# Retention core of a three-layer kernel: head-on-partition inputs, gapped scans, k decay on GpSimd, two sets of score banks

## The chip, the core and the metric

The kernel runs on one core of a Trainium2 chip. That core has five engines with instruction queues of their own: PE (TensorE, matrix products), DVE (VectorE), ACT (ScalarE), POOL (GpSimd) and SP (SyncE, which here only issues transfers). They meet through semaphores. The time is that of one execution on the device in microseconds (us); lower is better.

## What is computed

Three layers in a row: a linear recurrence with decay (4 sequences, 8 heads, 768 tokens, head dimension 48), then two layers of mixture of experts. The change touches only the recurrence:

```python
state = np.zeros((B, H, D, D), dtype=np.float32)
for t in range(S):
    kt, vt, rt, wt = (k[:, :, t], v[:, :, t], r[:, :, t], w[:, :, t])
    cur = np.einsum('bhd,bhe->bhde', u[None] * kt, vt)
    y[:, :, t] = np.einsum('bhd,bhde->bhe', rt, state + cur)
    state = wt[:, :, :, None] * state + np.einsum('bhd,bhe->bhde', kt, vt)
```

The first expert layer sends each of the 3072 tokens (rows of 384 numbers) to one of 8 experts, `out[mask] = gate_w * (relu(x @ w1[e]) @ w2[e])`; the second sends each to two experts. w lies between 0.8 and 0.95.

## The kernel before

The recurrence goes in 24 steps, one for each chunk of 128 tokens of a sequence (6 chunks for each of 4 sequences, all 8 heads at once). `batches` (L318) makes of the first three sequences a hardware loop of six written-out steps, and writes the last six out behind it. What each engine does, and in which order, is written by hand in its own block; a step of number g takes its operands from the buffers of step g+1 or g-1 where the text below says so.

The recurrence within a chunk is turned into products: `rest` holds, for each head dimension, the product of the decays behind a token, and `grow` the reciprocal of the products from a token on. k times `rest` is `k_dec`, r times `grow` is `r_dec`. The scores of a head are k_dec by r_dec, masked with `causal` (L719); the output is scores by v (L1083) plus r_dec by the state from the chunks before (L1080), into one bank of PSUM; DVE adds the term of u, `bonus_v`, and writes `y_tok` (L741). The state for the next chunk is k_tok (k_dec transposed, L1061, and copied by ACT, L562) by v (L1070) plus the old state (L734), times the total decay (L736). The input comes with tokens on the 128 partitions, so PE transposes w, k and r of the next chunk (`turn`, L1018: twelve transposes of two heads each) into three PSUM banks, and DVE's `decay_step` (L676) reads them there: four scans for `rest` (L685), one for each pair of heads, a reciprocal, k_dec (L691), four scans for `grow` (L694), r_dec (L699).

The order of a step g on the engines:
- PE: scores (L1053), transposes of k_dec (L1061), `turn` for g+1 (L1026), state products (L1070), transposes of y_tok of step g-1 (L1034), output products (L1080 and L1083), gate products (L1042, after ACT has copied the transposed rows, L552).
- DVE: mask (two halves, L719), bonus (L724), `decay_step` of g+1, state_sum, state, y_tok.
- POOL: rk = r*k (L434), ruk = rk*u (L437), bonus_v (L441), each 128 x 384.
- ACT: k_tok, the copies for the gate, and the store of y_tok.
- SP: for chunk g+3, four loads of 192 KB with 48 floats in a row (L332, L334) once step g's output is done, and a store of zeros into the output (L345).

The expert layers (from L446, L570, L776, L1095 on) begin when the last y_tok is stored; their lines are the same before and after, but for their numbers.

## Time and profile before

| what | value |
|---|---|
| median of 3 runs | 1128.05 us |
| lowest and highest of them | 1124.4 and 1131.2 us |
| span of the profiled execution, first to last instruction | 1121.9 us |
| busy share of the span: PE, DVE, POOL, ACT | 88%, 50%, 32%, 26% |
| the recurrence, from the first transpose on PE to the last y_tok | about 8 to 200 us |
| the rest: routing and the first expert layer, gate, routing and the second | about 200 to 1120 us |

For the profiled execution the records give the span alone and no time of its own, so the span stands for it; the median is 6.15 us longer. The busy share of the whole span says nothing about the recurrence, which is 17% of it: there PE and DVE are both nearly always busy, which the stretches in the rows below show. PEclk is the granted clock of TensorE, 1.00 for 2.4 GHz and 0.50 for 1.2 GHz. Rows of a line give its count, its busy time, and the mean time of one.

### The profile page before, as it was taken

The numbers are of one execution on the slowest core, as the hardware profiler recorded it, in microseconds if no ns is written. First come the engines' busy times: TensorE is split into PE (matmuls) and PEld (weight loads), VectorE is DVE, ScalarE is ACT, GpSimd is POOL, SyncE is SP. The second block draws the span as 40 slices with busy tenths as digits, with TensorE's granted clock in tenths as the row PEclk, the third lists the DMA queues.
The fourth block names the chain that finished last, engine by engine and source line by source line (L and its number), as shares of the span: only waits on it lengthen the run. The fifth ranks groups of instructions, "written<-read, shape, count | busy, mean of one in ns | idle before, by whom it ended". The sixth has DMA issues, their size and how long they took to land.

```text
span 1121.9 us, 25632 instructions
## 1 busy us (share of the span) xinstructions
PE 984.0 (88%) x6268; PEld 883.5 (79%) x6269; DVE 564.7 (50%) x1120; ACT 294.0 (26%) x462; POOL 360.5 (32%) x440
## 2 busy tenths in 40 slices
PE   6999999359999999959138999999999999999995
PEld 5988998248888889848027888889889888889884
DVE  5998999754333233314885335353533535353331
ACT  1111111214222222214123233242422324242220
POOL 4333333324222222210253334243433424343222
PEclk9998999569999999988559999999999999999998
DMA  8667564331111111133304525252252425222222
GB/s 144 154 146 168 135 155 126 119 101 70 43 42 42 42 39 38 39 99 103 114 14 153 144 42 147 36 154 42 33 164 35 148 42 152 45 35 41 38 43 35
DMA packets 149662, 97.17 MB, mean 87 GB/s; under 512 B 114224, under 2 KB 140592, under 8 KB 149616
## 3 DMA queue, kind: packets, MB, share of 16 engines
q1 hardware_dynamic: 124096, 60.00, 19.2%
q0 software_dynamic: 14400, 31.55, 13.7%
q10 hardware_dynamic: 11120, 5.09, 1.6%
q8 instruction: 20, 0.33, 0.1%
q14 instruction: 26, 0.21, 0.1%
HBM read 71.79 MB, written 24.82 MB: 86 GB/s over the span
## 4 chain that ended last, share of the span: by engine, by line
PE 68%; DVE 9%; issue 2%; DMA 2%; ACT 1%; POOLq 0%; POOL 0%; DVEq 0%; SPq 0%; ACTq 0%
PE ps L1167 19%; PE ps L1169 19%; PE ps L1168 19%; PE ps L1188 6%; PE ps L1162 2%; DVE row_mix L940 1%; PE ps L1103 1%; PE ps L1114 1%; DVE low_hot L864 1%; DVE slot_cmp L875 1%; DMA stage<-in_moe_w_dram 1%; DMA sx<-moe_rows,src_now 1%; PE ps L1123 1%; DVE high_is L860 1%; DVE x_lo L947 1%
## 5 line engine op out<-in xcount | busy, mean ns | idle before, releaser
L952 DVE SCALAR_TENSOR_TENSOR hid_lo<-ps,hid_hi 128x512 fp32r<-128x512 f32 x154 | 106.3, 690 | 313.8 <-ACT hid_hi L632 309.9
L1167 PE MATMUL ps<-w_hi,hid_hi 128*128 x616 | 215.0, 349 | 5.0 <-issue 3.5
L1167 PE MATMUL ps<-w_hi,x_hi 128*128 (+1 forms) x462 | 199.1, 431 | 20.1 <-DVE x_lo L947 12.9
L1168 PE MATMUL ps<-w_lo,hid_hi 128*128 x616 | 207.9, 337 | 0.0
L1169 PE MATMUL ps<-w_hi,hid_lo 128*128 x616 | 207.8, 337 | 0.0
L1168 PE MATMUL ps<-w_lo,x_hi 128*128 (+1 forms) x462 | 185.4, 401 | 0.0
L1169 PE MATMUL ps<-w_hi,x_lo 128*128 (+1 forms) x462 | 185.3, 401 | 0.0
L627 ACT ACTIVATE h_tok<-ps 128x512 f32<-128x512 f32 x154 | 92.2, 599 | 314.6 <-PE ps L1169 275.4
L498 POOL DMA_INDIRECT out_dram<-sy,dst_now x52 | 92.7, 1783 | 211.9 <-DVE sy L963 202.8
L632 ACT ACTIVATE hid_hi<-ps 128x512 fp32r<-128x512 f32 x154 | 91.9, 597 | 250.2 <-PE ps L1188 245.0
L1167 PEld LDWEIGHTS ps<-w_hi,hid_hi 128*128 128x128 f32 x616 | 116.3, 189 | 10.1 <-issue 6.6
L1167 PEld LDWEIGHTS ps<-w_hi,x_hi 128*128 128x128 f32 x462 | 88.3, 191 | 42.3 <-issue 27.1
L1168 PEld LDWEIGHTS ps<-w_lo,hid_hi 128*128 128x128 f32 x616 | 116.3, 189 | 3.2
L1169 PEld LDWEIGHTS ps<-w_hi,hid_lo 128*128 128x128 f32 x616 | 116.0, 188 | 0.0
L1169 PEld LDWEIGHTS ps<-w_hi,x_lo 128*128 128x128 f32 x462 | 88.5, 192 | 21.7
L1168 PEld LDWEIGHTS ps<-w_lo,x_hi 128*128 128x128 f32 x462 | 88.9, 192 | 14.6
L1188 PE MATMUL ps<-ident,h_tok 128*128 128x128 f32 x616 | 92.4, 272 | 5.2 <-ACT h_tok L627 5.2
L1188 PEld LDWEIGHTS ps<-ident,h_tok 128*128 128x128 f32 x616 | 76.1, 140 | 12.7 <-ACT h_tok L627 7.4
L477 POOL DMA_INDIRECT sx<-moe_rows,src_now x55 | 56.3, 1023 | 44.1 <-POOL src_now L474 42.4
L495 POOL DMA_INDIRECT moe_rows<-sy,dst_now x25 | 26.4, 1055 | 137.0 <-DVE sy L960 137.0
L613 ACT ACTIVATE w_hi<-stage 128x1536 f32 (+1 forms) x40 | 58.7, 1478 | 5.8 <-DMA stage<-in_moe_w_dram 5.7
L945 DVE CAST x_hi<-ps 128x384 fp32r<-128x384 f32 x79 | 43.7, 553 | 31.6 <-PE ps L1162 31.6
(195 smaller groups left out, 1273.7 us busy)
## 6 DMA issues: line engine op xcount, KB each, us to landing
stage<-in_moe_w_dram SPq DMA_DIRECT2D x20, 1536.0 KB, 12.1
out_dram<-zeros SPq DMA_DIRECT2D x25, 192.0 KB, 3.7
w_in<-in_w_dram SPq DMA_DIRECT2D x24, 192.0 KB, 2.7
k_in<-in_k_dram SPq DMA_DIRECT2D x24, 192.0 KB, 3.3
r_in<-in_r_dram SPq DMA_DIRECT2D x24, 192.0 KB, 4.1
v_in<-in_v_dram SPq DMA_DIRECT2D x24, 192.0 KB, 4.2
x_rows<-y_tok ACTq DMA_DIRECT2D x24, 192.0 KB, 3.3
stage<-moe_rows SPq DMA_DIRECT2D x6, 768.0 KB, 4.6
```

The lines of the kernel that those rows point to most:

```text
L477: pool.indirect_dma_start(out=sx[u][:, 0:width], out_offset=None, in_=rows, in_offset=bass.IndirectOffsetOnAxis(ap=src_now[u][:, :].bitcas ...
L495: pool.indirect_dma_start(out=y_dram, out_offset=where, in_=sy[u][:, :], in_offset=None)\
L498: pool.indirect_dma_start(out=out, out_offset=where, in_=sy[u][:, 0:C], in_offset=None, compute_op=ALU.add).then_inc(s_scatter[l][u], 16)
L613: act.activation(hi[:, bass.ds((n % 2) * WSZ + at, HALF)], raw[:, at:at + HALF], ACT.Copy)\
L627: act.activation(h_tok[:, half * FC // 2:(half + 1) * FC // 2, :], h_ps[half], ACT.Copy)\
L632: act.activation(hid_hi[:, half * FC // 2:(half + 1) * FC // 2, :], hT_ps[half], ACT.Relu)\
L945: dve.tensor_copy(x_hi[:, :, :], sxT_ps).then_inc(s_xhi[l], 1)
L952: dve.scalar_tensor_tensor(hid_lo[:, part, :], hT_ps[half], 0.0, hid_hi[:, part, :], ALU.max, ALU.subtract).then_inc(s_hlo[l], 1)
L1167: pe.matmul(out_ps, hi, w_hi[:, bass.ds(at, width)], start=first, stop=False)
L1168: pe.matmul(out_ps, hi, w_lo[:, bass.ds(at, width)], start=False, stop=False)
L1169: return pe.matmul(out_ps, lo, w_hi[:, bass.ds(at, width)], start=False, stop=final)
L1188: last = pe.transpose(hT_ps[half][:, m, :], h_tok[:, half * FC // 2 + m, :], ident[:, :])
```

## The change

The host lays the inputs out in three arrays. w_T and kr_T have the head dimension first: 48 rows for the even heads (partitions 0 to 47) and 48 for the odd ones (64 to 111), tokens along the row, so `turn` and its three PSUM banks go; rkv keeps r, k and v with tokens on partitions, for rk, bonus_v and the products with v. SP issues five loads for a chunk where it issued four: two of 96 KB for w, two of 192 KB for k and r, one of 576 KB; 1152 KB in all for 768 KB.

`w_in` gets a gap of one zero between the four pairs of heads. A scan over all 516 columns, state = w*state + seed, starts anew in a gap, since the seed tile holds 1 there (or the reciprocal of the total) and 0 elsewhere: one scan (L717) takes the place of the four of L685, one (L729) that of the four of L694. Both inputs of each lie in SBUF. k_dec moves from DVE to POOL (L443), where rk and ruk of step g+1 now also come ahead of bonus_v of step g; their inputs lie in SBUF too. The multiplication of the state by the total decay moves from DVE (L736) to four activations on ACT into `carried` (L586), ahead of k_tok in ACT's order. The scores go in turn to banks 3, 4 and 0, 1, and one instruction masks all eight heads (L768). On PE the transposes of y_tok and the gate products come ahead of the state products. DVE fills the padding of the three input buffers before the first scan, and SP waits for that (`s_pad`).

`decay_step` and `turn` are taken out whole. The core of the rest:

```diff
+        w_in = [att_sb(f"w_in{i}", [P, WN + 1]) for i in range(NIN)]
+        kr_in = [att_sb(f"kr_in{i}", [P, 2, HP, P]) for i in range(NIN)]
+        tok_in = [att_sb(f"tok_in{i}", [P, 3, H, D]) for i in range(NIN)]
+        rest = [att_sb(f"rest{i}", [P, WN + 1]) for i in range(2)]
+        grow = att_sb("grow", [P, WN])
+        seed_back, seed_on = att_sb("seed_back", [P, WN + 1]), att_sb("seed_on", [P, WN])
...
+        kt_ps = bank(2, HP)
+        sc_ps = [[bank(3, HP), bank(4, HP)], [bank(0, HP), bank(1, HP)]]
+        sc_both = [ps[:, n:n + 2, :].rearrange("p n (a b) -> p (n a) b", a=HP) for n in (3, 0)]
...
             def load_chunk(b, c):
                 i = c % NIN
+                for par in range(2):
+                    rows = slice(HS * par, HS * par + D)
+                    sp.dma_start(w_in[i][rows, 1:WN + 1].rearrange("d (h t) -> d h t", t=W1)[:, :, 0:P],
+                                 w_T[b, c, par]).then_inc(s_win[i], 16)
+                for par in range(2):
+                    rows = slice(HS * par, HS * par + D)
+                    sp.dma_start(kr_in[i][rows, :, :, :], kr_T[b, c, par]).then_inc(s_krin[i], 16)
+                sp.dma_start(tok_in[i][:, :, :, :].rearrange("p a h d -> p (a h d)"), rkv[b, c])\
+                  .then_inc(s_tokin[i], 16)
...
-            def bonus_step(b, c, last):
+            def before_step(b, c):
                 g, i = b * NC + c, c % NIN
-                pool.wait_ge(s_in[i], 64 * (b * (NC // NIN) + c // NIN + 1))
-                pool.tensor_tensor(rk[:, :, :], r_in[i][:, :, 0:D], k_in[i][:, :, 0:D], ALU.mult).then_inc(s_rk, 1)
+                pool.wait_ge(s_krin[i], 32 * (b * (NC // NIN) + c // NIN + 1))
+                pool.wait_ge(s_rest, g + 1)
+                pool.wait_ge(s_y, g + 1)
+                pool.tensor_tensor(k_dec[c % 2][:, :, :], kr_in[i][:, 0, :, :],
+                                   rest[c % 2][:, 1:WN + 1].rearrange("p (h t) -> p h t", t=W1)[:, :, 1:W1],
+                                   ALU.mult).then_inc(s_kd, 1)
+                pool.wait_ge(s_tokin[i], 16 * (b * (NC // NIN) + c // NIN + 1))
+                pool.wait_ge(s_ruk, 1 + g)
+                pool.tensor_tensor(rk[:, :, :], tok_in[i][:, 0, :, :], tok_in[i][:, 1, :, :], ALU.mult)\
+                    .then_inc(s_rk, 1)
                 pool.wait_ge(s_rk, g + 1)
                 pool.wait_ge(s_bonus, 1 + g)
                 pool.tensor_tensor(ruk[:, :, :], rk[:, :, :], u_all[:, :].rearrange("p (h d) -> p h d", h=H),
                                    ALU.mult).then_inc(s_ruk, 1)
+            before_step(0, 0)
+            def bonus_step(b, c, last):
+                g, i = b * NC + c, c % NIN
+                if not last:
+                    before_step(b + (c + 1) // NC, (c + 1) % NC)
                 pool.wait_ge(s_bonus, 1 + g + 1)
                 pool.wait_ge(s_ytok, 1 + g)
-                pool.tensor_tensor(bonus_v[:, :, :], v_in[i][:, :, :],
+                pool.tensor_tensor(bonus_v[:, :, :], tok_in[i][:, 2, :, :],
                                    bonus[:, :].unsqueeze(2).to_broadcast([P, H, D]), ALU.mult).then_inc(s_bv, 1)
...
+                n = b * (NC - 1) + c
+                if c > 0:
+                    act.wait_ge(s_state, 1 + n)
+                    act.wait_ge(s_y, 2 + g)
+                    for h in range(HP):
+                        last_op = act.activation(carried[:, h, :], state[c % 2][:, h, :], ACT.Copy,
+                                                 scale=rest[c % 2][:, 1 + h * W1:2 + h * W1])
+                    last_op.then_inc(s_carry, 1)
                 if c < NC - 1:
-                    n = b * (NC - 1) + c
                     act.wait_ge(s_kt, n + 1)
-                    act.wait_ge(s_y, 1 + g)
+                    act.wait_ge(s_y, 2 + g)
                     act.activation(k_tok[:, :, :], kt_ps, ACT.Copy).then_inc(s_ktok, 1)
...
+            for i in range(NIN):
+                dve.memset(w_in[i][:, 1:WN + 1].rearrange("p (h t) -> p h t", t=W1)[:, :, 0:P], 1.0)
+                dve.memset(w_in[i][:, 0:WN + 1:W1], 0.0)
+                dve.memset(kr_in[i][:, :, :, :], 0.0).then_inc(s_pad, 1)
+                if i == 0:
+                    dve.memset(seed_back[:, 1:WN + 1].rearrange("p (h t) -> p h t", t=W1)[:, :, 0:P], 0.0)
+                    dve.memset(seed_back[:, W1:WN + 1:W1], 1.0)
+                    dve.memset(seed_on[:, :], 0.0).then_inc(s_seed, 1)
...
+            def suffix_products(b, c):
+                g, i = b * NC + c, c % NIN
+                dve.wait_ge(s_win[i], 32 * (b * (NC // NIN) + c // NIN + 1))
+                dve.tensor_tensor_scan(rest[c % 2][:, 1:WN + 1][:, ::-1], w_in[i][:, 1:WN + 1][:, ::-1],
+                                       seed_back[:, 1:WN + 1][:, ::-1], 1.0, ALU.mult, ALU.add).then_inc(s_rest, 1)
+            def inverse_totals(b, c):
+                dve.wait_ge(s_rest, b * NC + c + 1)
+                dve.reciprocal(seed_on[:, 0:WN:W1], rest[c % 2][:, 1:WN + 1:W1]).then_inc(s_inv, 1)
+            def inverse_suffixes(b, c):
+                g, i = b * NC + c, c % NIN
+                dve.wait_ge(s_inv, g + 1)
+                dve.tensor_tensor_scan(grow[:, :], w_in[i][:, 0:WN], seed_on[:, :], 1.0, ALU.mult, ALU.add)\
+                   .then_inc(s_grow, 1)
+            def decayed_r(b, c):
+                g, i = b * NC + c, c % NIN
+                dve.wait_ge(s_krin[i], 32 * (b * (NC // NIN) + c // NIN + 1))
+                dve.wait_ge(s_grow, g + 1)
+                dve.tensor_tensor(r_dec[c % 2][:, :, :], kr_in[i][:, 1, :, :],
+                                  grow[:, :].rearrange("p (h t) -> p h t", t=W1)[:, :, 0:P], ALU.mult)\
+                   .then_inc(s_rd, 1)
...
             def attention_step(b, c, last):
                 g = b * NC + c
-                dve.wait_ge(s_y, 1 + g)
-                for half in range(2):
-                    dve.wait_ge(s_sc, g * 2 + half + 1)
-                    dve.tensor_tensor(scores[half][:, :, :], sc_ps[half],
-                                      causal[:, :].unsqueeze(1).to_broadcast([P, H // 2, P]), ALU.mult)\
-                       .then_inc(s_scm, 1)
-                dve.wait_ge(s_ruk, g + 1)
-                dve.wait_ge(s_bv, 1 + g)
+                n = b * (NC - 1) + c
+                after = (b + (c + 1) // NC, (c + 1) % NC)
+                if not last:
+                    dve.wait_ge(s_y, 1 + g + 1)
+                    dve.wait_ge(s_carry, 1 + b * (NC - 1) + max(c - 1, 0))
+                    suffix_products(*after)
+                dve.wait_ge(s_sc, g + 1)
+                dve.tensor_tensor(scores[c % 2][:, :, :], sc_both[c % 2],
+                                  causal[:, :].unsqueeze(1).to_broadcast([P, H, P]), ALU.mult).then_inc(s_scm, 1)
+                if not last:
+                    inverse_totals(*after)
+                dve.wait_ge(s_ruk, 1 + g + 1)
+                dve.wait_ge(s_bv, 2 + g)
                 dve.tensor_reduce(bonus[:, :], ruk[:, :, :], AX.X, ALU.add).then_inc(s_bonus, 1)
                 if not last:
-                    decay_step(b + (c + 1) // NC, (c + 1) % NC, b * (NC - 1) + c)
+                    inverse_suffixes(*after)
                 if c < NC - 1:
-                    n = b * (NC - 1) + c
-                    ahead = rest[:, :, 0:1].to_broadcast([P, HP, 2 * D])
                     dve.wait_ge(s_st, n + 1)
                     if c == 0:
-                        dve.tensor_copy(state_sum[:, :, :], st_ps).then_inc(s_sum, 1)
+                        dve.tensor_copy(state[1][:, :, :], st_ps).then_inc(s_state, 1)
                     else:
-                        dve.tensor_tensor(state_sum[:, :, :], st_ps, state[c % 2][:, :, :], ALU.add).then_inc(s_sum, 1)
-                    dve.wait_ge(s_sum, 1 + n + 1)
-                    dve.tensor_tensor(state[(c + 1) % 2][:, :, :], state_sum[:, :, :], ahead, ALU.mult)\
-                       .then_inc(s_state, 1)
-                dve.wait_ge(s_y, 1 + g + 1)
-                dve.wait_ge(s_bv, 1 + g + 1)
+                        dve.wait_ge(s_carry, 1 + n)
+                        dve.tensor_tensor(state[(c + 1) % 2][:, :, :], st_ps, carried[:, :, :], ALU.add)\
+                           .then_inc(s_state, 1)
+                if not last:
+                    decayed_r(*after)
+                dve.wait_ge(s_y, 2 + g + 1)
+                dve.wait_ge(s_bv, 2 + g + 1)
                 dve.wait_ge(s_xst[c % 2], 16 + (b * (NC // 2) + c // 2) * 16)
                 dve.tensor_tensor(y_tok[c % 2][:, :], y_ps, bonus_v[:, :, :].rearrange("p h d -> p (h d)"),
                                   ALU.add).then_inc(s_ytok, 1)
...
             def attention_step(b, c, last_chunk):
                 g, i, par = b * NC + c, c % NIN, c % 2
                 n = b * (NC - 1) + c
-                pe.wait_ge(s_kd, 1 + g + 1)
+                pe.wait_ge(s_kd, g + 1)
                 pe.wait_ge(s_rd, 1 + g + 1)
-                pe.wait_ge(s_scm, 1 + g * 2)
+                pe.wait_ge(s_scm, g)
                 for h in range(H):
-                    last = pe.matmul(sc_ps[h % 2][:, h // 2, :], head_on(k_dec[par], h),
+                    last = pe.matmul(sc_ps[par][h % 2][:, h // 2, :], head_on(k_dec[par], h),
                                      head_on(r_dec[par], h), start=True, stop=True)
-                    if h >= H - 2:
-                        last.then_inc(s_sc, 1)
-                pe.wait_ge(s_xl, 1 + g)
+                last.then_inc(s_sc, 1)
                 if c < NC - 1:
                     pe.wait_ge(s_ktok, 1 + n)
                     for h in range(HP):
                         last = pe.transpose(kt_ps[:, h, :], k_dec[par][:, h, :], ident[:, :])
                     last.then_inc(s_kt, 1)
-                if not last_chunk:
-                    turn(b + (c + 1) // NC, (c + 1) % NC)
+                pe.wait_ge(s_xl, 1 + g)
+                pe.wait_ge(s_ytok, 1 + g)
+                gate_turn_x(c)
+                gate_product_x(g, c)
+                pe.wait_ge(s_tokin[i], 16 * (b * (NC // NIN) + c // NIN + 1))
                 if c < NC - 1:
                     pe.wait_ge(s_ktok, 1 + n + 1)
-                    pe.wait_ge(s_sum, 1 + n)
+                    pe.wait_ge(s_state, 1 + n)
                     for h in range(H):
                         lo, col = HS * (h % 2), D * (h % 2)
                         last = pe.matmul(st_ps[lo:lo + HS, h // 2, col:col + D], k_tok[:, h // 2, lo:lo + HS],
-                                         v_in[i][:, h, :], start=True, stop=True)
+                                         tok_in[i][:, 2, h, :], start=True, stop=True)
                     last.then_inc(s_st, 1)
-                pe.wait_ge(s_ytok, 1 + g)
-                gate_turn_x(c)
-                pe.wait_ge(s_scm, 1 + g * 2 + 2)
+                pe.wait_ge(s_scm, 1 + g + 1)
                 if c > 0:
-                    pe.wait_ge(s_state, 1 + n)
+                    pe.wait_ge(s_carry, 1 + n)
                 for h in range(HP):
                     if c > 0:
-                        pe.matmul(y_ps[:, 2 * h * D:2 * (h + 1) * D], r_dec[par][:, h, :], state[par][:, h, :],
+                        pe.matmul(y_ps[:, 2 * h * D:2 * (h + 1) * D], r_dec[par][:, h, :], carried[:, h, :],
                                   start=True, stop=True, skip_group_check=True)
                     for q in (2 * h, 2 * h + 1):
-                        last = pe.matmul(y_ps[:, q * D:(q + 1) * D], scores[q % 2][:, h, :], v_in[i][:, q, :],
+                        last = pe.matmul(y_ps[:, q * D:(q + 1) * D], scores[par][:, (q % 2) * HP + h, :], tok_in[i][:, 2, q, :],
                                          start=(c == 0), stop=True, skip_group_check=True)
                 last.then_inc(s_y, 1)
-                gate_product_x(g, c)
```

DVE, a step inside a sequence. Before, a step reads so:

```order
L719 TENSOR_TENSOR scores<-ps,causal 128x512
L718 REGISTER_ALU
L719 TENSOR_TENSOR scores<-ps,causal 128x512
L724 TENSOR_REDUCE bonus<-ruk 128x8
L685 SCALAR_TENSOR_TENSOR rest<-ps,ones 128x128 x4
L689 RECIPROCAL grow<-rest 128x4
L691 TENSOR_TENSOR k_dec<-ps,rest 128x512
L694 SCALAR_TENSOR_TENSOR grow<-ps,grow,ones 128x127 x4
L697 REGISTER_ALU
L699 TENSOR_TENSOR r_dec<-ps,grow 128x512
L734 TENSOR_TENSOR state_sum<-ps,state 128x384
L735 REGISTER_ALU
```

and after:

```order
L717 SCALAR_TENSOR_TENSOR rest<-w_in,seed_back 128x516
L768 TENSOR_TENSOR scores<-ps,causal 128x1024
L723 RECIPROCAL seed_on<-rest 128x4
L774 TENSOR_REDUCE bonus<-ruk 128x8
L729 SCALAR_TENSOR_TENSOR grow<-w_in,seed_on 128x516
L778 REGISTER_ALU
L783 TENSOR_TENSOR state<-ps,carried 128x384
L737 TENSOR_TENSOR r_dec<-kr_in,grow 128x512
L787 REGISTER_ALU
L790 TENSOR_TENSOR y_tok<-ps,bonus_v 128x384
```

The first scan now stands ahead of the mask, k_dec and one of the two state instructions are gone, and scans and r_dec read no PSUM.

POOL, two steps inside a sequence. Before:

```order
L434 TENSOR_TENSOR rk<-r_in,k_in 128x384
L437 TENSOR_TENSOR ruk<-rk,u_all 128x384
L439 REGISTER_ALU
L441 TENSOR_TENSOR bonus_v<-v_in,bonus 128x384
L434 TENSOR_TENSOR rk<-r_in,k_in 128x384
L437 TENSOR_TENSOR ruk<-rk,u_all 128x384
```

and after:

```order
L443 TENSOR_TENSOR k_dec<-kr_in,rest 128x512
L448 TENSOR_TENSOR rk<-tok_in 128x384
L452 TENSOR_TENSOR ruk<-rk,u_all 128x384
L464 TENSOR_TENSOR bonus_v<-tok_in,bonus 128x384
L441 REGISTER_ALU
L443 TENSOR_TENSOR k_dec<-kr_in,rest 128x512
```

k_dec, rk and ruk belong to step g+1, the bonus_v behind them to step g, whose y_tok waits for it.

PE, a step inside a sequence. Before:

```order
L1053 MATMUL ps<-r_dec,k_dec 128x128 x8
L1061 MATMUL ps<-ident,k_dec 128x128 x4
L1026 MATMUL ps<-ident,w_in 128x128 x4
L1026 MATMUL ps<-ident,k_in 128x128 x4
L1026 MATMUL ps<-ident,r_in 128x128 x4
L1066 REGISTER_ALU
L1070 MATMUL ps<-v_in,k_tok 64x48 x8
L1034 MATMUL ps<-ident,y_tok 128x128 x3
L1075 REGISTER_ALU
L1080 MATMUL ps<-state,r_dec 128x96
L1083 MATMUL ps<-v_in,scores 128x48 x2
```

and after:

```order
L1089 MATMUL ps<-r_dec,k_dec 128x128 x8
L1095 MATMUL ps<-ident,k_dec 128x128 x4
L1070 MATMUL ps<-ident,y_tok 128x128 x3
L1078 MATMUL ps<-gate_w,gxT 128x8 x3
L1103 REGISTER_ALU
L1107 MATMUL ps<-tok_in,k_tok 64x48 x8
L1115 MATMUL ps<-carried,r_dec 128x96
L1118 MATMUL ps<-tok_in,scores 128x48 x2
```

Twelve transposes are gone, and the gate products (L1078), which ended a step, stand right behind the transposes of the rows that they need.

## Rows read from the trace of the kernel before

**Rows 1.** Timeline: the line that writes y_tok (start, duration, engine, line).

```profile
23.29 0.55 DVE L741 TENSOR_TENSOR y_tok<-ps,bonus_v 128x384 f32<-128x384 f32 x1
...
116.79 0.55 DVE L741 TENSOR_TENSOR y_tok<-ps,bonus_v 128x384 f32<-128x384 f32 x1
...
124.26 0.55 DVE L741 TENSOR_TENSOR y_tok<-ps,bonus_v 128x384 f32<-128x384 f32 x1
...
199.37 0.56 DVE L741 TENSOR_TENSOR y_tok<-ps,bonus_v 128x384 f32<-128x384 f32 x1 [3.68 <-PE ps L1083]
```

**Rows 2.** Stretches: length, then busy time of each engine, PEclk, DMA share, GB/s.

```profile
82.00:84.00 2.00, 1.92 (x20) 1.83 (x20) 1.97 (x5) 0.18 (x1) 0.18 (x1) 1.00 0.00 1
84.00:86.00 2.00, 2.00 (x19) 1.78 (x18) 1.45 (x4) 0.00 (x0) 0.00 (x0) 0.53 0.88 164
22.00:202.00 180.00, 172.82 (x1759) 162.90 (x1758) 166.23 (x384) 29.65 (x69) 62.10 (x67) 0.94 0.61 146
```

**Rows 3.** Timeline of PE and ACT in the step behind 119 us.

```profile
119.04 0.67 PE L1070 MATMUL ps<-v_in,k_tok 128*64 128x48 f32 x16
...
119.64 0.55 PE L1034 MATMUL ps<-ident,y_tok 128*128 128x128 f32 x3
...
120.03 0.36 PE L1080 MATMUL ps<-state,r_dec 128*128 128x96 f32 x2
...
120.23 0.49 ACT L552 ACTIVATE gxT<-ps 128x384 f32<-128x384 f32 x1 [1.56 <-PE ps L1034]
...
122.64 0.80 PE L1042 MATMUL ps<-gate_w,gxT 128*128 128x8 f32 x6
...
123.55 1.16 PE L1053 MATMUL ps<-r_dec,k_dec 48*128 48x128 f32 x16
...
124.64 0.66 PE L1061 MATMUL ps<-ident,k_dec 128*128 128x128 f32 x4
...
125.14 0.60 PE L1026 MATMUL ps<-ident,w_in 128*128 128x128 f32 x4
```

**Rows 4.** Groups of instructions by line, 0 to 300 us, DVE: busy, mean ns.

```profile
L694 DVE TENSOR_TENSOR_SCAN grow<-ps,grow,ones 128x127 f32<-128x127 f32 x96 | 38.1, 459 | 0.0
...
L685 DVE TENSOR_TENSOR_SCAN rest<-ps,ones 128x128 f32<-128x128 f32 x96 | 32.6, 401 | 7.6 <-PE ps L1026 7.6
...
L699 DVE TENSOR_TENSOR r_dec<-ps,grow 128x512 f32<-128x512 f32 x24 | 16.6, 691 | 0.8
...
L691 DVE TENSOR_TENSOR k_dec<-ps,rest 128x512 f32<-128x512 f32 x24 | 15.9, 662 | 0.0
...
L811 DVE TENSOR_TENSOR_SCAN seen<-ps,ones 128x24 f32<-128x24 f32 x8 | 0.9, 182 | 0.2 <-PE ps L1142 0.2
```

**Rows 5.** The same view, POOL.

```profile
L434 POOL TENSOR_TENSOR rk<-r_in,k_in 128x384 f32<-128x384 f32 x24 | 24.0, 1001 | 1.4 <-DMA v_in<-in_v_dram 1.4
...
L441 POOL TENSOR_TENSOR bonus_v<-v_in,bonus 128x384 f32<-128x384 f32 x24 | 19.9, 829 | 120.0 <-DVE bonus L724 120.0
...
L461 POOL TENSOR_TENSOR w_lo<-stage,w_hi 128x1536 f32 x1 | 3.5, 3519 | 7.2 <-ACT w_hi L613 7.2
```

**Rows 6.** Timeline behind the recurrence: POOL and DVE at once, then DVE alone.

```profile
220.59 3.65 POOL L461 TENSOR_TENSOR w_lo<-stage,w_hi 128x1536 fp32r<-128x1536 f32 x1
...
220.97 3.58 DVE L875 TENSOR_TENSOR slot_cmp<-slot_cmp,has 128x280 f32<-128x280 f32 x1
...
236.08 0.45 DVE L875 TENSOR_TENSOR slot_cmp<-slot_cmp,has 128x280 f32<-128x280 f32 x1
```

**Rows 7.** Timeline of PE at the lower clock.

```profile
60.19 2.08 PE L1053 MATMUL ps<-r_dec,k_dec 48*128 48x128 f32 x16 [1.27 <-DVE r_dec L699]
...
197.86 0.71 PE L1080 MATMUL ps<-state,r_dec 128*128 128x96 f32 x2
...
199.14 1.20 PE L1042 MATMUL ps<-gate_w,gxT 128*128 128x8 f32 x5
```

**Rows 8.** Timeline: DVE's first instruction.

```profile
2.00 0.38 DVE L672 MEMSET y_tok<- 128x384 f32 x1 [1.88 <-issue]
```

117 lines of the change are left out of this document (43 added, 74 removed).

## Prediction

> **What bounds the kernel now.** I read the timeline for the steps, then the stretches, then the groups and single waits inside a step. The recurrence makes its 24 outputs between 23.29 and 199.37 us, 23 intervals of 7.66 us on average; inside a sequence an undisturbed one takes 7.47 us [rows 1]. From 22 to 202 us PE is busy for 172.8 of 180 us and DVE for 166.2, POOL for 62.1, and the granted clock is 0.94 of 2.4 GHz [rows 2]. So two engines bound a step at once, and a change that relieves only one gains little. This one relieves both: twelve transposes on PE (the first four start at 125.14, 0.50 us behind the transposes of k_dec [rows 3]; the twelve take 3 x 0.44 = 1.3 us), k_dec (0.66 us [rows 4]) and one 384-wide instruction on DVE. The expert layers are the same before and after, and the SP queue does not issue their weights before the routing. All of the change lies in those 23 intervals and in the first.
>
> **DVE alone.** A scan of 24 columns takes 0.18 us and one of 128 takes 0.40 [rows 4]: 2.1 ns a column and 0.13 fixed, so 516 columns take an estimated 1.22 us, against 4 x 0.34 = 1.4 for the four. By the second kind (127 columns, 0.46 us [rows 4]) it is up to 2.69 ns a column, 1.5 us; I take 1.22, since the new scans have a constant as their first value, as the 0.40 has. Mask 1.2, r_dec 0.69, the state sum 0.55, y_tok 0.55 and the small ones come to some 6.2 us a step. DVE alone would go from 7.4 to 6.2.
>
> **PE alone.** From the starts in [rows 3]: scores 1.09, transposes of k_dec 0.50, of y_tok 0.39. Now the gate products stand right behind these and must wait for ACT: its copy starts 0.59 us behind the start of the transposes and takes 0.49, and with the hand-over back the wait ends some 1.23 us behind that start. In the old order the state and output products covered it. Then gate products 0.80, state products 0.60, output products 2.61. Sum: 1.09 + 0.50 + 1.23 + 0.80 + 0.60 + 2.61 = 6.8; 6.9 with one more hand-over. PE alone would bound a step at 6.9. ACT's four new multiplications (under 1 us, by the 0.49 of a copy four times as wide) lie at the step's start, four us ahead of the output products, and cost nothing; they would if ACT came to k_tok over 2 us late.
>
> **POOL, and what it shares with DVE.** k_dec on POOL: 384 columns take 1.00 us and 1536 take 3.52 [rows 5], 2.19 ns a column, so 512 take 1.28. POOL then needs 1.28 + 1.00 + 1.00 + 0.83 = 4.1 us a step and alone bounds nothing. But: a DVE instruction with both inputs in SBUF that takes 0.45 us by itself took 3.58 when it started at 220.97, while POOL worked on two SBUF inputs from 220.59 to 224.24 [rows 6]. 224.24 and the rest of 0.45 is 224.55, when it ended. It waited for the whole of POOL's instruction. Before the change this touches nothing in the recurrence: the scans, k_dec and r_dec read PSUM. Now both scans and r_dec read two SBUF tiles, and all four of POOL's instructions do. The Trainium skill states this rule ("SBUF - State Buffer", Who interferes with whom): a DVE instruction with two SBUF inputs and a GpSimd one that reads SBUF hold the shared port for their whole length, whichever comes first. It speaks against this change, and the 3.58 us agree.
>
> So they go one behind the other, and they also depend on each other in a ring: rest scan 1.22, k_dec 1.28, rk 1.00, grow scan 1.22 (DVE gets there in time, it then waits), ruk 1.00, r_dec 0.69 (which waits for the end of ruk), bonus_v 0.83 (which waits for r_dec), y_tok 0.55, and the next rest scan stands behind y_tok on DVE. Sum 7.79; instructions of one engine overlap at their ends by some 0.08 (the 1.00 + 0.83 + 1.00 of before stand that close), so I take 7.4, with 7.2 and 8.0 (scan at 1.5) as bounds. The wait that is added for POOL thus lands on r_dec, and behind r_dec are queued y_tok on DVE and the scores of the next step on PE: PE idles some 0.5 us there. At an undisturbed clock the step goes from 7.47 to 7.4: nearly all that DVE and PE save is lost.
>
> **The clock.** At about 84.1 us the granted clock falls to 1.2 GHz, though PE was busy for 1.92 of the 2 us ahead (84 to 86: 0.53) [rows 2]. What ran there was output products and gate products alone; it came back once scores and transposes had run. The same happens after an idle PE at the turn from one sequence to the next, as ahead of 60.19 us [rows 7]. In the old step the output and gate products take 3.4 of 7.47 us. In the new one the stretch without scores and transposes is the ACT wait 0.7, gate 0.8, state 0.6, output 2.6 and the wait for r_dec 0.5: 5.2 of 7.4 us. It holds more idle time, and the transposes are what is removed. At the low clock a step costs: scores 2.05 for 1.09 [rows 7, 3]; output products 1.28 us for each pair of heads (197.86 to 199.14 [rows 7]), 5.1 in all; the rest, 2.3 us at full clock, times 1.8 as the scores, 4.1; the ACT wait 0.7: 12.0 us, PE-bound. With a share x of steps' worth of low clock the mean step is 7.4(1 - x) + 12.0x. In the old kernel the mean clock of 0.94 means x near 0.12. I estimate 0.3 for the new one, since the stretch of the kind that preceded a fall is one and a half times as long: 8.78 us. This is the weakest number here; 0.1 and 0.5 are its ends (7.86 and 9.70).
>
> **Start, end, transfers.** DVE first fills 3 x 1541 + 1036 columns and the two old fills, some 6.4 us at 1 ns a column (0.38 for 384 at 2.00 [rows 8]), so the first scan starts near 8.5 us; the ring of the first step and the gate products, now ahead of its output, take back what that gains. At the end the last step's gate products are already done. Together -1 us, between -3 and +2. The loads grow from 768 to 1152 KB a chunk, but in pieces of 512 bytes and more for 192; three chunks are held, so a load has over a step to land, and I take nothing.
>
> **Sum.** 23 x 8.78 = 201.9 for 176.1 us, +25.8; -1: +24.8. The span goes from 1121.9 to 1146.7; the median stood 6.15 us above the span, so 1153 us.
>
> **The rivals.**
> - *The ring holds, and the clock does as before.* The gaps of PE stay short, and the five low stretches of before cost the same. 23 x (7.4 - 7.47) = -1.6, -1: 1125 us, 1121 to 1133 with the ring between 7.2 and 7.7. For it: the new gaps are 0.5 to 0.7 us, half of the 1.27 ahead of 60.19 [rows 7]. Against it: the fall at 84 us had no gap ahead. The Trainium skill ("TensorE: Matmul & The Clock Gate", HAM oscillation) names long idle gaps of PE as what brings the clock down; by that alone this rival would win, but the fall at 84 us disagrees.
> - *DVE and POOL do not block each other as long as I think* (scans may leave gaps to POOL, which the row of [rows 6], a plain product, does not show), and the clock holds: PE bounds at 6.9. 23 x (6.9 - 7.47) = -13.1, -1: 1114 us, faster. It decides once the ring falls under 6.9.
> - *The clock stays low nearly throughout:* 12 us a step, +100, 1227 us. Against it: a step still has 2 us of scores and transposes in a row, 3.6 at the low clock, like that which brought the clock back.
> - *Loads land late*, DVE waits for w at a step's head: half a us a step, 1140. The store of zeros and 5 loads share the queue; against it is the depth of three chunks.
>
> **How the numbers follow.** Forecast 55%; first rival 20%, second 17%, low throughout 4%, loads 4%. With x between 0.1 and 0.5 the forecast spans 1131 to 1174; the range takes in the first rival and the upper half of the second's, 1113 to 1176. About 0.5% (5.6 us) is what a measurement can tell from no change. Faster: the second rival and a fifth of the first, 0.21. Same: the rest of the first and the lowest of the forecast, 0.18. Slower: 0.61.
>
> **What would show it.** Blocking: DVE's grow scan (L729) and r_dec (L737), or POOL's ruk and bonus_v, show two lengths, with and without the other's; if L729 always takes 1.2 us and L452 1.0, it fell. Clock: the mean granted clock between 22 and 202 us under 0.9; over 0.93, the first or second rival. PE alone: gate products (L1078) wait for ACT in each step. Steps of y_tok: 7.4 us undisturbed, 10 to 12 with low clock. The forecast is wrong if undisturbed steps take under 7.1 us, or if there are no more low stretches than before.

## The result, and the profile after

| what | before | after |
|---|---|---|
| median (4 runs each) | 1126.32 us | 1214.72 us |
| lowest and highest | 1124.4 and 1131.2 us | 1213.45 and 1218.21 us |
| span of the profiled execution | 1121.9 us | 1213.8 us |
| first to last y_tok, 23 intervals | 176.1 us | 263.0 us |

The ratio is 1.080 with a 95% interval of 1.076 to 1.085. The change makes the kernel 8% slower. The forecast was 1153 us with a range up to 1176: right in its sign, far too small in its size, and what came is close to the rival to which it gave 4%.

The stretches say where the time went. The columns are those of [rows 2]: length, busy time of PE, PE's weight loads, DVE, ACT and POOL, granted clock, DMA share, GB/s. First before, the recurrence and all behind it:

```profile
22.00:199.37 177.37, 170.76 (x1752) 161.31 (x1751) 163.97 (x375) 29.29 (x67) 62.10 (x67) 0.94 0.62 147
199.37:1121.90 922.53, 802.26 (x4442) 712.12 (x4442) 389.86 (x718) 262.32 (x391) 288.23 (x333) 0.93 0.28 74
```

and after:

```profile
22.00:290.38 268.38, 250.46 (x1518) 232.27 (x1518) 134.54 (x179) 52.72 (x148) 106.28 (x89) 0.60 0.44 132
...
290.38:1213.80 923.42, 801.42 (x4436) 712.26 (x4436) 391.49 (x718) 262.06 (x390) 288.74 (x333) 0.93 0.28 74
```

Behind the last y_tok nothing moved: 923.4 us for 922.5. In the recurrence DVE is busy for 134.5 us in place of 164.0, as the change wants it. PE has 234 matmuls fewer in the records and is busy 80 us longer. It is busy for 93% of the stretch, so this is no kernel that waits. It is a kernel whose matmuls are slow: the granted clock is at the lower of its two levels. Two more stretches of the kernel after:

```profile
30.00:60.00 30.00, 27.98 (x174) 25.89 (x172) 15.28 (x22) 6.14 (x17) 13.32 (x12) 1.00 0.50 150
74.00:260.00 186.00, 172.83 (x1032) 160.26 (x1030) 96.42 (x126) 36.78 (x102) 77.05 (x64) 0.50 0.46 136
```

From 74 to 260 us the clock is 0.50 without a break. For 30 to 60 us the column says 1.00, and that isn't so: the rate of matmuls is that of the second row (5.8 and 5.5 a us), and a step's scores, 1.16 us at the full clock [rows 3], take 2.08:

```profile
39.22 2.08 PE L1089 MATMUL ps<-r_dec,k_dec 48*128 48x128 f32 x16
```

The column shows the full clock until the first change on record, here at 70.67 us. By the lengths of the matmuls the clock was low from 22 to about 67 us, so the true mean of the long stretch is an estimated 0.52 and not 0.60. A clock column is to be read together with the length of a known instruction.

One whole step at that clock, on PE, with the two y_tok of DVE that frame it (start, duration, engine, line; in brackets the idle time ahead and what ended it):

```profile
131.20 2.08 PE L1089 MATMUL ps<-r_dec,k_dec 48*128 48x128 f32 x16
131.31 0.56 DVE L790 TENSOR_TENSOR y_tok<-ps,bonus_v 128x384 f32<-128x384 f32 x1 [4.12 <-PE ps L1118]
...
133.21 1.11 PE L1095 MATMUL ps<-ident,k_dec 128*128 128x128 f32 x4
...
134.12 0.85 PE L1070 MATMUL ps<-ident,y_tok 128*128 128x128 f32 x3
...
135.64 1.42 PE L1078 MATMUL ps<-gate_w,gxT 128*128 128x8 f32 x6 [0.67 <-ACT gxT L575]
...
136.99 1.10 PE L1107 MATMUL ps<-tok_in,k_tok 128*64 128x48 f32 x16
...
138.02 0.74 PE L1115 MATMUL ps<-carried,r_dec 128*128 128x96 f32 x2
...
143.30 1.44 PE L1089 MATMUL ps<-r_dec,k_dec 48*128 48x128 f32 x10
...
143.52 0.56 DVE L790 TENSOR_TENSOR y_tok<-ps,bonus_v 128x384 f32<-128x384 f32 x1 [4.23 <-PE ps L1118]
```

From scores to scores 12.10 us: scores 2.01, transposes of k_dec 0.91, transposes of y_tok and the wait for ACT 1.52, gate products 1.35, state products 1.03, output products 5.28. PE has 0.67 us of idle time in it. DVE waits 4.23 us for PE. The groups of the first 300 us (count, busy, mean ns, idle time ahead) say the same of all steps, where [rows 4, 5] stand for before:

```profile
L1118 PE MATMUL ps<-tok_in,scores 128*128 128x48 f32 x384 | 91.5, 393 | 0.0
...
L1078 PE MATMUL ps<-gate_w,gxT 128*128 128x8 f32 x150 | 34.3, 351 | 23.3 <-ACT gxT L575 23.3
...
L729 DVE TENSOR_TENSOR_SCAN grow<-w_in,seed_on 128x516 f32<-128x516 f32 x24 | 33.3, 1388 | 0.0
...
L717 DVE TENSOR_TENSOR_SCAN rest<-w_in,seed_back 128x516 f32<-128x516 f32 x24 | 30.1, 1254 | 0.3 <-issue 0.2
...
L443 POOL TENSOR_TENSOR k_dec<-kr_in,rest 128x512 f32<-128x512 f32 x24 | 29.5, 1229 | 152.0 <-DVE rest L717 152.0
...
L790 DVE TENSOR_TENSOR y_tok<-ps,bonus_v 128x384 f32<-128x384 f32 x24 | 13.4, 558 | 91.1 <-PE ps L1118 91.1
```

L1118 takes 393 ns where the same products in e1_gap16, below, take 273. All of DVE's idle time ahead of y_tok, 91 us, is put down to PE.

### The profile page after: what moved, and what is told of

It is laid out like the page before. It is cut to its first block, busy times and chain, and to the rows that moved or that the text cites. A ratio compares the mean times of both kernels' runs of the same rounds, so it can differ in the third digit from the quotient of the medians.

```text
span 1213.8 us, 25053 instructions
## 1 busy us (share of the span) xinstructions
PE 1056.5 (87%) x5980; PEld 948.5 (78%) x5981; DVE 540.8 (45%) x920; ACT 317.1 (26%) x542; POOL 409.4 (34%) x454
## 4 chain that ended last, share of the span: by engine, by line
PE 83%; DVE 8%; issue 3%; DMA 3%; ACT 2%; ACTq 1%; SPq 0%; POOLq 0%; POOL 0%; DVEq 0%
PE ps L1201 18%; PE ps L1202 17%; PE ps L1203 17%; PE ps L1118 6%; PE ps L1222 5%; PE ps L1089 4%; PE ps L1115 3%; PE ps L1078 3%; PE ps L1196 2%; PE ps L1095 2%; PE ps L1107 2%; PE ps L1070 1%; DVE row_mix L989 1%; ACT gxT L575 1%; PE ps L1137 1%
## 5 line engine op out<-in xcount | busy, mean ns | idle before, releaser
L1118 PE MATMUL ps<-tok_in,scores 128*128 128x48 f32 x384 | 91.5, 393 | 0.0
L1118 PEld LDWEIGHTS ps<-tok_in,scores 128*128 128x128 f32 x384 | 90.1, 327 | 0.4
L443 POOL TENSOR_TENSOR k_dec<-kr_in,rest 128x512 f32<-128x512 f32 x24 | 29.5, 1229 | 152.0 <-DVE rest L717 152.0
```

Source lines behind the costliest of these rows:

```text
L1118: last = pe.matmul(y_ps[:, q * D:(q + 1) * D], scores[par][:, (q % 2) * HP + h, :], tok_in[i][:, 2, q, :], start=(c == 0), stop=True, skip ...
```

## The theories

**Theory A:** the loss is PE's clock, and PE's own work sets it: the transposes that the change took away, or the old order of the rest, had kept it up. **Rival B:** the loss comes from the ring of DVE and POOL and from the new waits; the clock goes with it, but PE's own work doesn't steer it. The two are far apart on one point: by A, giving PE *more* to do can make the kernel faster; by B it can only make it slower.

Then, within A: is it the transposes (T), PE's wait for ACT ahead of the gate products (W), or the place of these products (P)?

All measured times stand here. "Recurrence" is the time from the first to the last y_tok of the profiled execution, and the clock that of 22 us to its last y_tok. The ratio is to the kernel before in runs on the same chip. A median is of 2 to 10 executions, a recurrence of one only, and that one need not be typical: the profiled execution of gap8 is the fastest of its four (1138.3 us), that of f_last12 the slowest of its ten (1125.5 us). In six of the runs the column has the fault shown above at the start, until the first change on record; with the lengths of the matmuls in its place, the means are the estimates behind the sign "~".

| run | median us | ratio, 95% | recurrence us | clock |
|---|---|---|---|---|
| after | 1214.7 | 1.080 (1.076-1.085) | 263.0 | 0.60, ~0.52 |
| e1_gap16 | 1129.1 | 1.005 (1.002-1.007) | 177.9 | 0.96 |
| e2_head16 | 1192.2 | 1.061 (1.056-1.067) | 238.0 | 0.81 |
| e3_gate_last | 1139.5 | 1.013 (1.009-1.017) | 190.6 | 0.78, ~0.76 |
| e4_warm | 1214.7 | 1.080 (1.073-1.087) | 260.8 | 0.51 (60 to 260) |
| b_drop8 | 1188.8 | 1.057 (1.053-1.062) | 191.0 | 0.82, ~0.80 |
| b_gate_early2 | 1167.9 | 1.035 (1.027-1.044) | 221.9 | 0.80 |
| gate_mid | 1156.3 | 1.027 (1.020-1.034) | 206.4 | 0.74, ~0.69 |
| swap_turns | 1181.8 | 1.052 (1.046-1.059) | 226.6 | 0.62, ~0.58 |
| gap8 | 1145.8 | 1.022 (1.014-1.029) | 187.6 | 0.86 |
| f_last8 | 1120.5 | 0.996 (0.994-0.999) | 170.7 | 0.95, ~0.92 |
| f_last12 | 1120.9 | 0.998 (0.996-1.001) | 173.0 | 0.94 |
| f_last8_thin | 1112.6 | 0.990 (0.988-0.993) | 164.6 | 0.92 |

## More work on PE, 85 us less time

The edit of e1_gap16, in PE's step of the kernel after:

```diff
                 gate_turn_x(c)
+                for h in range(16):
+                    pe.transpose(sc_ps[1 - par][0][:, h % HP, :], k_dec[par][:, h % HP, :], ident[:, :])
                 gate_product_x(g, c)
```

> The kernel after, with 16 more transposes a step on PE, between the transposes of y_tok and the gate products, where PE waits for ACT; their results go into a free score bank and are not used. PE gets more to do and nothing else changes. Theory A (the twelve transposes that the change took away were what kept the granted clock up; without them PE runs at 1.2 GHz through the recurrence and is the bound there): the clock comes back to 0.9 and more, a step falls from 11.4 to some 7.7 us, 1120 to 1145 us in all, faster than the kernel after by some 85 us though it does more. Rival B (the 90 us come from the ring of DVE and POOL and the new waits, and the clock only accompanies them, or doesn't depend on what PE does): the 16 cost 0.23 us each at the low clock (4 take 0.91 in the step behind 131 us), 3.7 us a step less the 0.67 us of idle time that they fill: 3.0 x 24 = +72, some 1286 us at a clock of 0.50.

```profile
22.00:205.37 183.37, 181.21 (x1888) 174.37 (x1888) 142.37 (x179) 48.86 (x148) 113.97 (x89) 0.96 0.66 194
```

The records hold 370 matmuls more than in the kernel after, and PE is busy for 69 us less with all of them. The median falls by 85.6 us, from 1214.7 to 1129.1. Rival B, which gave 1286, is out. Most steps of e1_gap16 inside a sequence take 7.5 to 7.8 us. In its timeline the wait for ACT is filled (L1101 are the added ones):

```profile
139.64 0.49 PE L1070 MATMUL ps<-ident,y_tok 128*128 128x128 f32 x3
...
139.97 1.91 PE L1101 MATMUL ps<-ident,k_dec 128*128 128x128 f32 x16
...
141.72 0.79 PE L1078 MATMUL ps<-gate_w,gxT 128*128 128x8 f32 x6
```

The three transposes of y_tok take 0.49 us where the kernel after needs 0.85, the gate products 0.79 for 1.42.

In e4_warm the addition stands once, ahead of the first chunk:

```diff
+            for h in range(60):
+                pe.transpose(sc_ps[1][0][:, h % HP, :], ident[:, :], ident[:, :])
+
             def gate_turn_x(c):
```

> The kernel after with 60 transposes of the identity at PE's start, while it waits for the first inputs: PE meets the first chunk at the high clock. Nothing in the steps changes. If the kernel after is slow because it starts at the low clock and never gets out of it, while it could stay at the high one (rival E): the clock stays up through the recurrence and the time falls to 1125 us. If the work of a step itself can't hold the high clock (theory A): it falls within the first two steps and stays at 0.50, 1208 to 1216 us.

```profile
22.00:60.00 38.00, 35.98 (x244) 33.54 (x243) 19.22 (x26) 7.49 (x22) 15.39 (x14) 0.56 0.56 160
60.00:260.00 200.00, 185.47 (x1118) 171.54 (x1118) 105.69 (x139) 40.74 (x112) 84.49 (x71) 0.51 0.46 138
```

The first interval of y_tok takes 9.7 us for 12.0, and the second is already at 12.2. The time is that of the kernel after. So the low clock isn't left over from a bad start: it comes back under the work of the steps.

## Is it the number of transposes, or the place?

e2_head16 has the same 16 transposes, but right behind the scores:

```diff
+                for h in range(16):
+                    pe.transpose(sc_ps[1 - par][0][:, h % HP, :], k_dec[par][:, h % HP, :], ident[:, :])
                 if c < NC - 1:
                     pe.wait_ge(s_ktok, 1 + n)
```

> The same 16 unused transposes a step, but right behind the scores, next to the transposes of k_dec; the gap where PE waits for ACT stays. It tells whether the amount of transposes in a step decides, or where they stand. If the amount alone decides (theory A1): as the run with the 16 in the gap, 1120 to 1145 us. If the rest of the step (gap, gate, state and output products) must be broken up or kept short too (theory A2, which I hold): the clock stays low in most of the steps, the recurrence takes 250 to 285 us, 1200 to 1240 us in all. Rival B (no influence on the clock): 16 x 0.23 x 24 = +88, 1303 us.

It took 1192 us, 8 us under the range of theory A2. Nearly all its intervals take between 9.1 and 11.4 us, so that each step is at the low clock for a part. The number alone doesn't decide: 16 in one place give back 85 us, in another 22. But the two runs differ in a second thing. PE's wait for ACT is filled in e1_gap16 (from 22 us to the last y_tok 1.8 us in 2 waits) and stays in e2_head16 (21.2 us in 23), so place and filled wait are not told apart here.

The opposite test is e3_gate_last, with no added work:

```diff
                 gate_turn_x(c)
-                gate_product_x(g, c)
                 pe.wait_ge(s_tokin[i], 16 * (b * (NC // NIN) + c // NIN + 1))
...
                 last.then_inc(s_y, 1)
+                gate_product_x(g, c)
```

> The kernel after with the gate products moved back to the end of a step on PE, as before the change: the wait for ACT is gone, PE has no idle time inside a step, and no work is added. Theory A (the clock follows what PE does, the idle time counts for it): some of the steps come back to the high clock, mean clock between 60 and 280 us at 0.6 to 0.8, 1160 to 1200 us. Rival C (only the removed transposes count, idle time doesn't): the clock stays at 0.50, and the gain is the idle time alone, 0.67 us x 23 = 15 us: 1198 us. Rival D (the idle time alone is what brings the clock down, as the rule on idle gaps has it): the clock is up throughout, 1125 us.

```profile
22.00:216.19 194.19, 177.94 (x1501) 165.65 (x1501) 138.41 (x179) 49.98 (x147) 113.74 (x89) 0.78 0.61 183
```

1139.5 us lies 20 below the range of theory A (1160 to 1200), and rivals C (1198) and D (1125) are out. Moving the three gate products of a step, which also takes away the wait in front of them, gives back 75 of 88 us. Eleven of the 23 intervals are at 7.1 to 7.7 us and the rest between 8.2 and 11.2: the clock goes up and down. Even at its high clock this kernel has an idle PE in each step, now ahead of the state products, where ACT's k_tok is waited for:

```profile
146.15 0.67 PE L1106 MATMUL ps<-tok_in,k_tok 128*64 128x48 f32 x16 [0.96 <-ACT k_tok L592]
```

## The same two edits in the kernel before

If the missing transposes and the new order are both causes, each must also hurt the kernel that had neither. b_drop8 takes eight of the twelve transposes away:

```diff
-                for src, dst, done, read in ((w_in, w_ps, s_wT, s_decay), (k_in, k_ps, s_kT, s_kd),
-                                             (r_in, r_ps, s_rT, s_rd)):
+                for src, dst, done, read in ((w_in, w_ps, s_wT, s_rd),):
...
-                dve.wait_ge(s_kT, g + 1)
-                dve.tensor_tensor(k_dec[i][:, :, :], k_ps, rest[:, :, 1:P + 1], ALU.mult).then_inc(s_kd, 1)
+                dve.tensor_tensor(k_dec[i][:, :, :], w_ps, rest[:, :, 1:P + 1], ALU.mult).then_inc(s_kd, 1)
```

and the same for r_dec.

> The kernel before with the eight transposes of k and r left out of each step: DVE takes k_dec and r_dec from the transposed w in their place, so that only w is transposed (the decayed k and r are wrong by that, and the rest of the program does the same work). DVE, POOL, ACT, the loads and all other products are as before. PE has 0.9 us a step less to do. Theory A (the transposes hold the granted clock up): the clock falls to 0.8 or less between 22 and 202 us and the kernel is slower with less work, 1135 to 1165 us. Rival B (the transposes are only work, and the loss of the changed kernel comes from its order and waits): DVE bounds at 7.4 us a step, 1118 to 1124 us.

```profile
22.00:215.32 193.32, 177.92 (x1584) 165.00 (x1583) 164.69 (x375) 29.31 (x67) 62.06 (x67) 0.82 0.58 136
215.32:1189.00 973.68, 815.86 (x4495) 723.51 (x4495) 430.85 (x737) 297.57 (x419) 328.93 (x343) 0.92 0.32 90
```

The total can't be used: the expert layers take 973.7 us for 922.5, which I had not foreseen. Their data come out of a recurrence whose values were changed; that tokens go to other experts is the likely reason, which no run shows. The recurrence can be used: 191.0 us for 176.1, at a clock of 0.82 for 0.94, with 0.9 us a step less to do on PE and the same instructions on DVE. Rival B said no slower. It is slower by 14.9 us. The loss sits at the start and at the turns of the sequences: six intervals take 9.7 to 11.7 us, the other seventeen 6.4 to 8.1, most of them the 7.5 of the kernel before. With eight transposes fewer most steps inside a sequence kept the high clock. And PE has more idle time as well (15.4 us for 6.6), most of it waits for k_tok (6.8 us) and for r_dec (4.3). So fewer transposes and more idle time come together here, and the run doesn't tell which of them costs the 15 us.

b_gate_early2 keeps all transposes and moves only the order:

```diff
                 if c < NC - 1:
                     pe.wait_ge(s_ktok, 1 + n + 1)
+                pe.wait_ge(s_ytok, 1 + g)
+                gate_turn_x(c)
+                gate_product_x(g, c)
+                if c < NC - 1:
                     pe.wait_ge(s_sum, 1 + n)
...
-                pe.wait_ge(s_ytok, 1 + g)
-                gate_turn_x(c)
                 pe.wait_ge(s_scm, 1 + g * 2 + 2)
...
                 last.then_inc(s_y, 1)
-                gate_product_x(g, c)
```

> The kernel before, all twelve transposes kept, with the transposes of y_tok and the gate products ahead of the state products, as the change has them; nothing else changes. It adds a wait of some 0.8 us for ACT to a PE that was busy for 172.8 of 180 us. Theory W, in its strong form (the order alone brings the clock down, as the 16 transposes behind the scores in e2_head16 did not mend it): 1160 to 1200 us at a clock of 0.85 or less in the recurrence. Rival T (the removed transposes are the cause, the order is harmless): the wait alone, 23 x 0.7 = +16, 1138 us at a clock of 0.94.

```profile
22.00:246.95 224.95, 209.35 (x1762) 196.54 (x1761) 167.86 (x375) 29.25 (x67) 62.02 (x67) 0.80 0.49 117
```

and of its timeline the wait that it adds:

```profile
121.69 0.81 PE L1042 MATMUL ps<-gate_w,gxT 128*128 128x8 f32 x6 [0.67 <-ACT gxT L552]
```

The time, 1167.9 us, lies in the range of theory W. The recurrence goes from 176.1 to 221.9 us, +45.9. From 22 us to the last y_tok PE is idle for 9.0 us more (15.6 for 6.6) and busy for 38.6 us more with the same products (209.4 for 170.8): most of the loss is the clock. So the order that the change gives PE, with the wait that comes with it, costs the old kernel 3.5% with not one instruction changed.

Put side by side, by the recurrence: the order costs 46 us in the old structure (221.9 for 176.1). In the new one, twelve transposes more and the gate products last give 173.0 (f_last12, below), the gate products last without transposes 190.6, and the kernel after has 263.0. So without transposes the order costs 72 us there, and with the gate products last the transposes are worth 18. With transposes in the wait the order costs 5: 177.9 in e1_gap16 for 173.0 in f_last12, and these are 16 transposes for 12. So the two don't simply add, and what the order costs depends on where the transposes stand. In b_gate_early2 all twelve were there, behind the scores, and didn't help.

## Is it PE's wait for ACT?

Two kernels take the wait away inside a sequence and leave the gate products ahead of the output products. gate_mid:

```diff
                 gate_turn_x(c)
-                gate_product_x(g, c)
...
                     last.then_inc(s_st, 1)
+                gate_product_x(g, c)
                 pe.wait_ge(s_scm, 1 + g + 1)
```

> The kernel after with the gate products between the state products and the output products. No work is added. They still come ahead of the output products, but no longer wait for ACT, since k_tok's copy and the state products cover that; at the low clock PE has then no idle time in a step, as in e3_gate_last. Theory W (PE's wait for ACT in front of the gate products, together with the missing transposes, is what keeps the clock low): most steps come back, 1130 to 1160 us. Rival P (what counts is that gate, state and output products follow each other without a scores or a transpose in between ahead of y_tok): the clock stays at 0.50, and only the idle 0.67 us x 23 go, 1198 us.

swap_turns puts the transposes of k_dec into the wait (and turns ACT's two copies round to match):

```diff
+                pe.wait_ge(s_xl, 1 + g)
+                pe.wait_ge(s_ytok, 1 + g)
+                gate_turn_x(c)
                 if c < NC - 1:
                     pe.wait_ge(s_ktok, 1 + n)
                     for h in range(HP):
                         last = pe.transpose(kt_ps[:, h, :], k_dec[par][:, h, :], ident[:, :])
                     last.then_inc(s_kt, 1)
-                pe.wait_ge(s_xl, 1 + g)
-                pe.wait_ge(s_ytok, 1 + g)
-                gate_turn_x(c)
                 gate_product_x(g, c)
```

> The kernel after with the transposes of y_tok ahead of those of k_dec, and ACT's copies in the same order: the four transposes of k_dec now fill most of the wait for ACT, and the gate products cover ACT's k_tok. Nothing is added. At the low clock the four take 0.91 us and the wait was 0.67, so no idle time is left; at the high one some 0.3 us. Theory W: 1130 to 1160 us. Rival P: 1198 us. Rival T (only the number of transposes in a step counts): the clock stays at 0.50, 1198 us too.

```profile
22.00:253.90 231.90, 226.59 (x1518) 212.53 (x1518) 137.60 (x179) 52.39 (x148) 108.42 (x89) 0.62 0.52 153
```

and a step of its timeline, without a wait:

```profile
121.95 1.06 PE L1101 MATMUL ps<-ident,k_dec 128*128 128x128 f32 x4
...
122.83 1.42 PE L1081 MATMUL ps<-gate_w,gxT 128*128 128x8 f32 x6
```

gate_mid came out at 1156 us, within what theory W said. swap_turns took 1182: 25 us more and 22 outside theory W, although PE has no idle time around that step (busy for 226.6 of 231.9 us in all). Rivals P and T, which gave 1198 and a clock that never rises, don't fit either: seven of its intervals are at 6.4 to 8.4 us. So both are faster than the kernel after (by 58 and 33 us), and among kernels without the wait the order of the same products still moves the recurrence by 36 us: 190.6, 206.4 and 226.6 us for the gate products at the end, in the middle and in front. Idle time of PE doesn't order them either. swap_turns, the slowest, has the least (5.3 us from 22 us to the last y_tok), e3_gate_last and gate_mid have 16.3 and 15.3. Each of the two edits removes the wait and changes the order at once, so that the wait by itself costs clock is argued and not shown. What property of the order matters is open. None of the three theories gives the three numbers.

gap8 is the smaller dose in the kernel after:

```diff
                 gate_turn_x(c)
+                for h in range(8):
+                    pe.transpose(sc_ps[1 - par][0][:, h % HP, :], k_dec[par][:, h % HP, :], ident[:, :])
                 gate_product_x(g, c)
```

> As e1_gap16 with 8 unused transposes in the wait for ACT in place of 16. 16 made PE the bound of a step, at 7.7 us; 8 take 0.96 us less. If 8 hold the clock as well, the ring of DVE and POOL bounds at 7.1 to 7.3 us, 1115 to 1120 us. If they hold it only in a part of the steps, which I hold to be likelier: 1130 to 1160 us.

1145.8 us (single executions between 1138 and 1155), as I held likelier: the clock is held in a part of the steps (0.86 in the fastest of them).

## The ring, at a clock that lets it show

f_last8 joins the two remedies: gate products at the end, and eight unused transposes in the 0.96 us that PE waits for k_tok.

```diff
                 gate_turn_x(c)
-                gate_product_x(g, c)
+                for h in range(8):
+                    pe.transpose(sc_ps[1 - par][0][:, h % HP, :], k_dec[par][:, h % HP, :], ident[:, :])
...
                 last.then_inc(s_y, 1)
+                gate_product_x(g, c)
```

> The kernel after with the gate products at the end of the step, as in e3_gate_last, and with 8 unused transposes behind those of y_tok, in the 0.96 us that PE waits there for ACT's k_tok. In e3_gate_last a step at the high clock took 7.1 to 7.25 us. 8 transposes take 0.96 us at the high clock (16 take 1.91) and so fit the wait. If the clock now stays up: 23 x 7.15 = 164 us of recurrence for 176 of the kernel before, 1108 to 1116 us, faster than both. If the eight are too few: low stretches as in e3_gate_last, 1125 to 1140 us.

f_last12 differs in one number:

```diff
-                for h in range(8):
+                for h in range(12):
```

> As f_last8 with 12 unused transposes, as many as the change took away. They take 1.44 us, 0.5 more than the wait has room for. If 8 already hold the clock, the 0.5 us a step show: 1118 to 1126 us. If 8 don't and 12 do, this one is the faster.

f_last8 takes 1120.5 us, 94 less than the kernel after and 0.996 of the kernel before (0.994 to 0.999): at best half a percent faster than where the change began. That is 4 us above the range of its forecast, 1108 to 1116. Most intervals are the expected 7.1 to 7.3 us, but the first of a sequence takes up to 10.2, and low stretches remain (clock ~0.92). Twelve transposes give 1120.9 us, in their expected range and the same as eight within the error; the 0.5 us a step that four more should cost doesn't show in the medians (its recurrence, 173.0 for 170.7, is that of the slowest execution).

In a step of f_last8 the two engines that share the work read so:

```profile
133.23 0.56 DVE L790 TENSOR_TENSOR y_tok<-ps,bonus_v 128x384 f32<-128x384 f32 x1 [0.90 <-POOL bonus_v L464]
...
135.01 1.19 POOL L443 TENSOR_TENSOR k_dec<-kr_in,rest 128x512 f32<-128x512 f32 x1 [1.99 <-DVE rest L717]
...
136.15 1.01 POOL L448 TENSOR_TENSOR rk<-tok_in 128x384 f32<-128x384 f32 x1
...
136.49 1.76 DVE L729 TENSOR_TENSOR_SCAN grow<-w_in,seed_on 128x516 f32<-128x516 f32 x1
...
137.24 1.80 POOL L452 TENSOR_TENSOR ruk<-rk,u_all 128x384 f32<-128x384 f32 x1
...
138.62 0.97 DVE L737 TENSOR_TENSOR r_dec<-kr_in,grow 128x512 f32<-128x512 f32 x1
...
139.00 1.28 POOL L464 TENSOR_TENSOR bonus_v<-tok_in,bonus 128x384 f32<-128x384 f32 x1
...
140.37 0.56 DVE L790 TENSOR_TENSOR y_tok<-ps,bonus_v 128x384 f32<-128x384 f32 x1 [0.78 <-PE ps L1119]
```

The ring is in it: y_tok at 133.23 waited for bonus_v, POOL then works without a break from k_dec to the end of the next bonus_v at 140.28, and the next y_tok starts 0.09 behind that, 7.14 us after the last one. PE has no idle time in this step either: the ring and PE bound it together.

The scan is issued at 136.49, while rk runs until 137.16, and ends at 138.25: 1.09 behind rk's end, about its own length. ruk is issued at 137.24 and ends at 139.04, 0.79 behind the scan. Each takes its turn. f_last8_thin cuts rk and ruk to one head, and takes the sum of bonus from u_all (ruk's cut is shown):

```diff
-                pool.tensor_tensor(ruk[:, :, :], rk[:, :, :], u_all[:, :].rearrange("p (h d) -> p h d", h=H),
+                pool.tensor_tensor(ruk[:, 0:1, :], rk[:, 0:1, :], u_all[:, :].rearrange("p (h d) -> p h d", h=H)[:, 0:1, :],
```

> f_last8 with POOL's rk and ruk on one head of eight (128 x 48 for 128 x 384), and the sum of bonus taken from u_all: the bonus term is wrong by that, nothing else of the recurrence changes. It measures what POOL and DVE do to each other. If they exclude each other (theory A's ring): the grow scan L729 goes from 1.75 us inside a step to 1.16 to 1.22, r_dec L737 from 0.97 to 0.55 to 0.7; the ring falls by some 1.6 us to 5.6, and PE bounds a step at some 7.0 us, so the time hardly falls. If the lengths of before are those of the scans and of r_dec themselves: they stay at 1.75 and 0.97. This one's time behind the recurrence can shift by a few us, since tokens go to other experts.

```profile
126.57 1.22 DVE L729 TENSOR_TENSOR_SCAN grow<-w_in,seed_on 128x516 f32<-128x516 f32 x1
...
126.80 1.07 POOL L452 TENSOR_TENSOR ruk<-rk,u_all 128x48 f32<-128x48 f32 x1 [0.42 <-DVE bonus L774]
127.83 0.82 POOL L464 TENSOR_TENSOR bonus_v<-tok_in,bonus 128x384 f32<-128x384 f32 x1
...
128.16 1.05 DVE L737 TENSOR_TENSOR r_dec<-kr_in,grow 128x512 f32<-128x512 f32 x1
```

The scan falls from 1.76 to 1.22 us (means of the 24: 1634 and 1223 ns). ruk, 48 columns, takes 1.07 where rk, as wide, takes 0.29: it ends 0.08 us behind the scan, for which it waited. r_dec did not fall as expected (1.05 for 0.97), because bonus_v now comes ahead of it: it ends 0.56 behind bonus_v's end. That part of the expectation had the order of the two wrong, not the blocking. The step is 6.8 to 7.0 us, PE's own time, as expected.

This also settles the rival that scans leave room to POOL: in these rows they don't.

## The prediction, step by step

**What bounds the kernel.** That all of the change lies in the recurrence is right. 87.0 of the 91.9 us of span lie between the first and the last y_tok, 4.1 ahead of it, 0.9 behind. In the kernel after PE alone bounds, as the forecast has it for a low step.

**DVE alone, PE alone, POOL.** The scan of 516 columns was put at 1.22 us: 1.22 measured (L717, and L729 without POOL). k_dec on POOL at 1.28: 1.23. ACT's four multiplications at no cost: they take 1.18 us, and no step waits for them in the kernel after. The wait of the gate products for ACT was there in each step (23.3 us in all), as said; 0.67 us at the low clock against the 0.7 of the sum.

**Blocking and ring.** The mechanism is confirmed by f_last8_thin. The size was a little high: where the clock is up (e3_gate_last, f_last8), steps take 7.1 to 7.25 us for the 7.4 of the sum; its lower bound was 7.2. In the kernel after the ring doesn't decide, since PE at 12 us a step is far behind it.

**The low step.** 12.0 us was the forecast, term by term 2.05 for the scores, 5.1 for the output products, 4.1 for the rest and 0.7 for the wait. Measured 12.0 to 12.2, from 2.01, 5.28, 4.14 and 0.67. The last step of a sequence, which has no state products, takes 10.0.

**The share of it. This is the step that failed.** The mean step is 11.44 us for 8.78. The share x of low clock was taken at 0.3 with 0.1 and 0.5 as its ends. By the prediction's own formula, 7.4(1 - x) + 12.0x, the measured 11.44 makes it 0.88, and by the lengths of the matmuls it is nearly 1 (the formula takes no account of the last steps of a sequence, which need only 10). The clock rises twice, around 67 and around 262 us, and is low again by 70.7 and 265.2. The value of 0.3 had no working behind it. The mean clock of 0.94 gives 0.12 as a share of the time, which is 0.08 as a share of steps of 7.4 and 12.0 us; and one and a half times 0.12 is 0.18. So the working leads further from the truth than the guess did, and that the step failed is a matter of its mechanism: it treats the falls as accidents that come somewhat more often with a longer stretch. That isn't how it goes. e4_warm falls within two steps from a high start, and the steps then stay low. The argument against "low throughout", that scores and transposes of 3.6 us in a row at the low clock would bring it back, was taken from steps of the old kernel in which twelve transposes more stood behind them. In the kernel after that block is scores 2.0, k_dec 0.9, y_tok 0.85. Both rises come behind such a block, but in the steps from 74 to 260 us the same block brings nothing back. Why the clock stays down there, in terms of what PE does, is open; what the runs show is that 16 transposes in the wait bring it to 0.96, and the gate products at the end of the step to ~0.76.

23 x (11.44 - 8.78) = 61 us of the miss of 61.7. The rest nearly cancels. The start was +4.1 us where -1 stood for start and end (5.1 worse), the stretch behind is 0.9 longer, and the median lies 0.9 us above the span where 6.15 had been added (5.2 less). That 6.15 wasn't a property of the kernel: in every run with both numbers on record an execution takes 1.7 to 1.8 us more than its span, so the profiled execution of before was, by estimate, some 4 us faster than the median. A part of the start is a wait that the prediction missed, in step 0, whose gate products now stand ahead of its output:

```profile
21.17 1.42 PE L1078 MATMUL ps<-gate_w,gxT 128*128 128x8 f32 x6 [4.72 <-ACT gxT L575]
```

They also need gate_w and the other small loads, which arrive in this time; which of the two it was, ACT or a load, wasn't tested. With the gate products last (e3_gate_last) the first y_tok comes at 25.59 us for 27.34, and the same order added 1.7 us to it in b_gate_early2, so this wait is worth some 1.8 of the 4.1 us. The rest of them is open.

**The rivals.** Clock as before (20%): fell. e1_gap16, at 1129 us, comes near its 1125, but with PE at 7.7 us a step as the bound and not the ring. No blocking (17%): fell, by f_last8_thin. Loads late: fell, DVE waited 0.3 us in all ahead of L717. Low throughout (4%, 1227 us): came, 12 us above the truth. It and the late loads had the least weight of all, 4% each.

**The page's rule.** In the kernel after PE is busy for 172.8 of 186 us at a clock of 0.50, with idle gaps of 0.67 us inside a sequence and at most 1.9 in its last step, and in swap_turns for 226.6 of 231.9 at ~0.58. The Trainium skill ("TensorE: Matmul & The Clock Gate", HAM oscillation) puts such a fall down to long idle gaps; the traces disagree, as the fall at 84 us [rows 2] had already. In b_gate_early2 the clock fell together with an added wait of 0.67 us, but there the order changed too. The Trainium skill's rule on the shared port ("SBUF — State Buffer", Who interferes with whom), a DVE instruction with two SBUF inputs against a GpSimd one that reads SBUF, holds for scans as well: the 516 columns took 1.76 us behind POOL's rk and 1.22 without it.

## What to carry over

Taking work off TensorE can cost time, where PE bounds and its clock depends on what it does. Before such a change, look in the trace of before for stretches at the lower clock under a busy PE. If there is even one, work out the step at the high and at the low clock, and don't put the low one at a few per cent. If the result is slow, put unused transposes into PE's waits as a test: it is one line, and if the time falls, the clock was the cause. That it doesn't fall says less: behind the scores the same 16 gave back only 22 us. Then try the same products in another order, those that wait for another engine at the end of the step first: here that alone gave back 75 of 88 us. Why it does isn't known, so it has to be measured and can't be counted on.

## What was not expected of the hardware

- A PE that is busy for 93% of the time stayed at 1.2 GHz for 186 us on end (0.50 from 74 to 260 us), on steps in which products of 8 to 96 columns take 7.7 of 12.1 us, and 16 more transposes a step, in PE's wait, brought it to 0.96.
- The order of the same PE work, with no wait inside a sequence at the low clock in any of the three, gave recurrences of 191, 206 and 227 us, and the slowest had the least idle time.
- Twelve and eight added transposes in f_last gave the same time. The 0.96 us that PE waits for k_tok without them cover two thirds of the 1.44 us that twelve take.
- The clock column can read 1.00 over 40 us of low clock when no change of it was recorded ahead.
